# Sparse attention and a rational MLP on one core: how q, k and V are cast, loaded and ordered

## What is computed

```
scores = (q @ k^T) / sqrt(64)
mask_local   = (rel >= 0) & (rel < 32)                 # heads 0-3, rel = query - key
mask_strided = (rel >= 0) & (key % 32 == query % 32)   # heads 4-7
attn = softmax(where(mask, scores, -1e9)); y = attn @ v
x = y.transpose(0, 2, 1, 3).reshape(4608, 512)
h = x @ w_in                                           # 512 -> 2048
g = (a0 + a1 h + a2 h^2 + a3 h^3) / (1 + |b0| |h| + |b1| h^2 + 1e-6)
out = g @ w_out                                        # 2048 -> 512, float32
```

## Time and profile before

| | |
|---|---|
| median of 3 runs | 556.41 us (552.62 to 563.49) |
| profiled execution | 551.65 us, its span 549.9 us |
| busy time PE / DVE / ACT | 353.3 / 345.4 / 255.2 us of the span |
| DMA packets | 176,959, of them 164,384 under 512 B; 60.35 MB |
| software queue q0 (POOL: casts, weights, stores) | 43,840 packets, 27.79 MB |
| hardware queue q1 (SP: loads, transposes) | 133,088 packets, 32.11 MB |

### The profile page before, as it was taken

One profiled execution on the slowest core, in us unless ns is written; L12 is line 12 of the kernel. 1 busy time (PEld: TensorE's weight loads), 2 busy tenths in 40 slices (PEclk: granted clock), 3 DMA queues, 4 the chain that ended last, 5 costly groups with the idle time before them and its releaser, 6 DMA issues.

```text
span 549.9 us, 7027 instructions
## 1 busy us (share of the span) xinstructions
PE 353.3 (64%) x2993; PEld 162.9 (30%) x3040; DVE 345.4 (63%) x286; ACT 255.2 (46%) x249; POOL 95.9 (17%) x104
## 2 busy tenths in 40 slices
PE   0010123355662996898479677999998769988763
PEld 0000112113221442444134333344443323333221
DVE  2000013012885795899449758799998996999920
ACT  0010001021735473666707516768847865788500
POOL 9400000050041061514301600010020110100100
PEclk9999999995955797998859967999999989999888
DMA  9999992799299999999994986442261211010101
GB/s 133 119 91 101 184 137 58 131 176 92 46 164 160 160 164 186 194 185 175 186 121 88 161 163 138 87 104 63 61 139 31 60 62 39 38 39 19 57 29 49
DMA packets 176959, 60.35 MB, mean 110 GB/s; under 512 B 164384, under 2 KB 173600, under 8 KB 176416
## 3 DMA queue, kind: packets, MB, share of 16 engines
q1 hardware_dynamic: 133088, 32.11, 40.9%
q0 software_dynamic: 43840, 27.79, 37.5%
HBM read 42.83 MB, written 25.95 MB: 125 GB/s over the span
## 4 chain that ended last, share of the span: by engine, by line
DVE 31%; PE 22%; DMA 16%; SPq 14%; ACT 10%; issue 5%; POOL 0%; DVEq 0%; POOLq 0%
PE ps_h L649 10%; DMA ptL<-pL 8%; PE ps_out L691 7%; SPq L433 6%; DVE u L668 6%; DVE z L676 4%; DMA xt<-xs 4%; SPq L442 4%; DMA xs<-xS 3%; DVE z L674 3%; DVE h L678 3%; ACT u L671 3%; DVE u L666 3%; ACT u L669 3%; DVE z L664 3%
## 5 line engine op out<-in xcount | busy, mean ns | idle before, releaser
L691 PE MATMUL ps_out<-Wout,h 128*128 128x512 bf16 x557 | 144.0, 410 | 24.5 <-ACT os L696 19.3
L649 PE MATMUL ps_h<-xt,Win 128*128 128x512 bf16 x548 | 137.7, 396 | 27.1 <-DMA xt<-xs 12.7
L653 ACT ACTIVATE h<-ps_h 128x512 bf16<-128x512 f32 x144 | 84.9, 597 | 79.8 <-PE ps_h L649 79.8
L691 PEld LDWEIGHTS ps_out<-Wout,h 128*128 128x128 bf16 x576 | 57.0, 104 | 101.5 <-ACT os L696 23.2
L649 PEld LDWEIGHTS ps_h<-xt,Win 128*128 128x128 bf16 x576 | 50.7, 101 | 96.5 <-ACT h L653 32.2
L702 POOL DMA_DIRECT2D out_dram<-os x36 | 37.1, 1121 | 241.1 <-ACT os L696 230.5
L669 ACT ACTIVATE u<-u,consts 128x4096 bf16<-128x4096 bf16 x18 | 66.7, 3706 | 17.2 <-DVE u L668 17.0
L389 POOL DMA_DIRECT2D lq<-in_q_dram x16 | 37.4, 2381 | 206.4 <-DMA vL<-v 205.6
L671 ACT ACTIVATE u<-u 128x4096 bf16<-128x4096 bf16 x18 | 65.1, 3619 | 0.0
L696 ACT ACTIVATE os<-ps_out 128x512 f32<-128x512 f32 x36 | 21.5, 597 | 62.3 <-PE ps_out L691 62.2
L389 POOL DMA_DIRECT2D lk<-in_k_dram x16 | 46.7, 3005 | 0.0
(11 more groups left out here) (41 smaller groups left out, 352.7 us busy)
## 6 DMA issues: line engine op xcount, KB each, us to landing
out_dram<-os POOLq DMA_DIRECT2D x36, 256.0 KB, 3.3
v<-in_v_dram POOLq DMA_DIRECT2D x8, 576.0 KB, 12.1
vL<-v SPq DMA_DIRECT2D x32, 96.0 KB, 3.3
lq<-in_q_dram POOLq DMA_DIRECT2D x16, 144.0 KB, 12.1
lk<-in_k_dram POOLq DMA_DIRECT2D x16, 144.0 KB, 13.5
sq<-in_q_dram POOLq DMA_DIRECT2D x8, 288.0 KB, 7.1
sk<-in_k_dram POOLq DMA_DIRECT2D x8, 288.0 KB, 9.6
vS<-v SPq DMA_DIRECT2D x16, 144.0 KB
```

The costliest lines, as they stand in the source:

```text
L649: r = e.matmul(ph.t[:, :], Win[:, kk, f * 128:(f + 1) * 128], xt.t[:, kk, :], start=(kk == 0), stop=(kk == NK1 - 1))
L653: P.op("act", lambda e, f=f, ph=ph, h=h: e.activation(h.t[:, f % G, :], ph.t[:, :], AF.Copy), 0.53, key, r=[ph], w=[h])
L691: r = e.matmul(po.t[:, :], groups[g].t[:, j, m * 128:(m + 1) * 128], Wout[:, kk, :], start=(kk == 0), stop=(kk == NF - 1))
```

## The change

- Casts of q and k for all heads go in natural order into `q16` and `k16`, in rows of 1024 elements, one DMA for four heads (`bulk`). The pair-of-heads layout is gone.
- All heads are loaded by the transposes that put even positions on partitions 0 to 63 and odd ones on 64 to 127. For the local heads four SBUF copies per batch put the other half's data across, so that heads on either half of the partitions have both an even and an odd plane (`PRE`, `halves`, `planes`).
- A local score block of 64 queries becomes two of 32: the even queries and the odd ones. The keys are read from two planes, and the PSUM output is written with a step of two, so that the keys stay in natural order. The queries of a block of 64 then stand in the order even, odd; the mask, the strided heads' xs rows and `xt` follow that order, and ACT puts h back into natural order as it evicts the first layer.
- The local pairs are heads (0, 2) and (1, 3), and the units go L, S, S, L.
- The strided heads' V is cast by POOL straight into SBUF (`vS`); only the local heads' V goes through DRAM.
- casts(1) and the second weights wait for loads of batch 0; casts(b+2) stands behind attention(b) in the list. Keys of the loads and of the MLP are later. The planner doubles a DMA's planned time when another queue is busy.
- xs is written in runs of 2048 elements (4 KB).
- The last chunk's four output blocks take four PSUM banks, those of the attention's tiles.

```diff
+                at = max(dmafree[e], t + o.dur)
+                busy = any(v > at for k, v in dmafree.items() if k != e)
+                dmafree[e] = at + o.dma * (2 if busy else 1)
...
-    R_lqT = ring("lqT", 4, [128, S])
-    R_lkT = ring("lkT", 4, [128, S])
-    R_sqT = ring("sqT", 2, [128, SW])
-    R_skT = ring("skT", 2, [128, SW])
+    SC = S // 2
+    SW = HL * SC
+    PRE = 2 * SC
+    QW = 2 * PRE + 2 * SW
+    R_tq = ring("tq", 2, [128, QW])
+    R_tk = ring("tk", 2, [128, QW])
...
+        qs = 64 * jj + 2 * (qi % 32) + (qi % 64) // 32
+        ks = np.maximum(0, 64 * jj - STRIDE) + ki
+        d = qs - ks
...
+    def bulk(s_t, d_t, b, h0, nh, hd, t, key, after):
+        n = nh * S * D
+        c = 1024
+        P.op("pool", lambda e: e.dma_start(
+            bass.AP(tensor=d_t, offset=(b * hd + h0) * S * D, ap=[[c, n // c], [1, c]]),
+            bass.AP(tensor=s_t.tensor, offset=s_t.offset + (b * H + h0) * S * D, ap=[[c, n // c], [1, c]])),
+            2.75, key, w=[t], dma=1.4 * nh / 4, after=after)
+    halves = {t.name: [Tile(t.name + n) for n in "LSX"] for t in R_tq.tiles + R_tk.tiles}
+    def planes(j, idx):
+        if j == 0:
+            return PRE + idx * SC, PRE + SW * 2 + idx * SC
+        return idx * SC, PRE + (2 + idx) * SC
...
-        local(0)
-        bulk(q, sq, HL, T_sqk[b])
-        bulk(k, sk, HL, T_sqk[b])
-        bulk(v, vs, 0, T_v[b])
-        local(1)
+        for n in range(2):
+            for s_t, d_t, t in ((q, q16, T_q[b][n]), (k, k16, T_k[b][n])):
+                bulk(s_t, d_t, b, HL * n, HL, H, t, key, after)
+            if n == 0:
+                bulk(v, vs, b, 0, HL, HL, T_v[b], key, after)
+        vS = vS_of[b] = R_vS.next()
+        for x in range(2):
+            P.op("pool", lambda e, x=x: e.dma_start(
+                vS.t[64 * x:64 * x + SB, :, :, :].rearrange("t h g d -> t h (g d)"),
+                bass.AP(tensor=v.tensor, offset=v.offset + ((b * H + HL) * S + 8 * x) * D,
+                        ap=[[16 * D, SB], [S * D, HL], [1, 8 * D]])),
+                1.0, key, w=[vS], dma=0.6, after=after)
...
-        key = b * 576 - 700
+        key = b * 576 - 20 if b else -700
...
+        tq, tk = R_tq.next(), R_tk.next()
+        for n in range(2):
+            for t, d_t, dt_ in ((tq, q16, T_q[b][n]), (tk, k16, T_k[b][n])):
+                hf = halves[t.name][n]
+                hf.new()
+                P.op("sp", lambda e, t=t, d_t=d_t, n=n: e.dma_start_transpose(
+                    t.t[:, PRE + n * SW:PRE + n * SW + SW],
+                    d_t[b, HL * n:HL * n + HL, :, :].rearrange("h (c two) d -> (h c) (two d)", two=2)),
+                    1.3, key + 2 * n, r=[dt_], w=[hf], dma=1.5)
+        for t, z in ((tq, halves[tq.name][2]), (tk, halves[tk.name][2])):
+            z.new()
+            for x in range(2):
+                d0 = 0 if x else PRE + 2 * SW
+                s0 = 2 * PRE if x else PRE
+                P.op("sp", lambda e, t=t, x=x, d0=d0, s0=s0: e.dma_start(
+                    t.t[64 * x:64 * x + 64, d0:d0 + PRE], t.t[64 - 64 * x:128 - 64 * x, s0:s0 + PRE]),
+                    0.5, key + 1, r=[halves[t.name][0]], w=[z], dma=0.3)
...
-        for kind, idx in (("L", 0), ("S", 0), ("L", 2), ("S", 2)):
+        for kind, idx in (("L", 0), ("S", 0), ("S", 2), ("L", 1)):
...
+                        for qp in range(2):
+                            p0 = 64 * (jj % 2) + 32 * qp
+                            for j in range(2):
+                                even, odd = planes(j, idx)
+                                off = 64 * j * QW
+                                r = e.matmul(pst[p0:p0 + 32, j, KW * (jj // 2):KW * (jj // 2) + KW].rearrange(
+                                                 "p (c k) -> p k c", k=2),
+                                             bass.AP(tensor=tq.t, offset=off + (even, odd)[qp] + 32 * jj,
+                                                     ap=[[QW, 64], [1, 32]]),
+                                             bass.AP(tensor=tk.t, offset=off + even + c0,
+                                                     ap=[[QW, 64], [odd - even, 2], [1, KW // 2]]),
+                                             start=False, stop=True, skip_group_check=True)
...
-                bass.AP(tensor=xs, offset=(b * S + par) * 256, ap=[[16 * 256, SB], [2 * 256, NBK], [1, 256]]),
+                bass.AP(tensor=xs, offset=(b * S + 32 * par) * 256, ap=[[64 * 256, SB // 4], [8 * 256, 4], [1, 8 * 256]]),
...
-        base = c * CH + 1150
+        base = c * CH + 1500 if c else 1000
...
-                P.op("act", lambda e, f=f, ph=ph, h=h: e.activation(h.t[:, f % G, :], ph.t[:, :], AF.Copy),
+                P.op("act", lambda e, f=f, ph=ph, h=h: e.activation(
+                    h.t[:, f % G, :].rearrange("p (j c k) -> p j k c", k=2, c=32),
+                    ph.t[:, :].rearrange("p (j k c) -> p j k c", k=2, c=32), AF.Copy),
...
-        base = c * CH + 1900
+        base = c * CH + 2250
+        last = [R_ps.next(), R_ps.next()] if c == NCH - 1 else None
         for m in range(CH // 128):
-            po = R_po.next()
+            po = last[m // 2] if last else R_po.next()
+            pot = po.t[:, m % 2, :] if last else po.t[:, :]
...
     casts(0)
     weights_in()
-    casts(1)
-    weights_out()
     nxt = 0
     st = loads(0)
+    casts(1, after=st["ops"])
+    weights_out(st["ops"])
     for b in range(B):
         cur = st
         if b + 1 < B:
             st = loads(b + 1)
+        xl = attention(b, cur)
         if b + 2 < B:
             casts(b + 2, after=st["ops"])
-        xl = attention(b, cur)
         gather(b, xl)
```

More of the change, by code:

```diff
@@ L380, in casts @@
+    def planes(j, idx):
+        if j == 0:
+            return PRE + idx * SC, PRE + SW * 2 + idx * SC
+        return idx * SC, PRE + (2 + idx) * SC
     def casts(b, after=()):
         key = b * 576 - 1500 if b > 1 else -1e5 + 3e4 * b
-        T_lqk[b][0].new()
-        T_lqk[b][1].new()
-        T_sqk[b].new()
+        for n in range(2):
+            T_q[b][n].new()
+            T_k[b][n].new()
         T_v[b].new()
[L387 to L392, removed]
@@ L418, in weights_out @@
                 w_out[512 * j:512 * j + 512, :].rearrange("(a p) n -> p a n", p=128)),
-                3.0, -4e4, w=[T_wout], dma=5.4)
+                3.0, -4e4, w=[T_wout], dma=5.4, after=after)
     def loads(b):
-        key = b * 576 - 700
+        key = b * 576 - 20 if b else -700
         st = {}
[L425 to L435, removed]
+        tq, tk = R_tq.next(), R_tk.next()
+        for n in range(2):
+            for t, d_t, dt_ in ((tq, q16, T_q[b][n]), (tk, k16, T_k[b][n])):
[13 more added lines that the diff above has]
+                    0.5, key + 1, r=[halves[t.name][0]], w=[z], dma=0.3)
+        hq, hk = halves[tq.name], halves[tk.name]
+        st["TL"] = [hq[0], hk[0], hq[2], hk[2]]
+        st["TS"] = [hq[1], hk[1]]
         vl = R_vL.next()
-        VB = (b * H) * S * D
+        VB = (b * HL) * S * D
         P.op("sp", lambda e: e.dma_start(
@@ L446, in loads @@
         st["vl"] = vl
[L447 to L456, removed]
+        st["vs"] = vS_of[b]
+        st["q"], st["k"] = tq, tk
+        st["ops"] = [vl.w[-1], hk[0].w[-1]]
         return st
@@ L478, in score @@
                     for jj in range(NQ):
[L479 to L482, removed]
[L483 to L484 removed]
+                        c0 = max(0, 32 * jj - 16)
+                        for qp in range(2):
[10 more added lines that the diff above has]
+                                             start=False, stop=True, skip_group_check=True)
                     return r
[L486 removed]
+                P.op("pe", score, 1.4, key, r=[T_c] + st["TL"], w=[sc])
                 flat = pst[:, :, 0:W].rearrange("p a (r c) -> p a r c", c=KW)
@@ L690, in mm @@
                         kk = g * G + j
-                        r = e.matmul(po.t[:, :], groups[g].t[:, j, m * 128:(m + 1) * 128], Wout[:, kk, :],
+                        r = e.matmul(pot, groups[g].t[:, j, m * 128:(m + 1) * 128], Wout[:, kk, :],
                                      start=(kk == 0), stop=(kk == NF - 1))
```

53 lines of the change are left out of this document (19 added, 34 removed).

## The result

The changed kernel takes 517.36 us (median of 4 runs, 514.78 to 520.31) against 557.48 us (4 runs, 552.62 to 563.49) for the kernel before: ratio 0.931, 95% interval 0.921 to 0.941. That is 40 us saved where 76 were forecast; the time lies inside the forecast range. The profiled execution took 515.17 us, its span 513.4.

What follows compares the result with a forecast made beforehand. VectorE was taken as the bound, kept idle early by SP's small packets waiting behind the casts' backlog. Prelude 95, stretch 363, tail 16.6 and 1.8 make 476, times 1.0086: 480 us, range 444 to 530.

Steps and rivals of the forecast that it cites:

- A burst keeps its bytes but loses 4608 small packets. I take 90% use: Stretch from VectorE's first to last MLP instruction: VectorE use rises from 84.5% to 90%, 386.6 to 363 us, -24.
- Eight first-layer tiles, 32 matmuls at 0.23 us ... near 10 us: 95: End of prelude: chunk 0's first-layer matmuls and an eviction take near 10 us, VectorE's first MLP instruction at 95 us.
- Queue starved still: Rival: bursts keep their bytes and SP waits as long; prelude 118, stretch 387, tail 16.6, scaled 528 us; 15%.
- 4600 more are 9 us: 85: Prelude: attention(0)'s packets left after the second burst (over at 76 us) take 9 us, to 85 us.
- The sign as written: Sign of being right, on SP: no issue over 10 us after the first 40 us.
- Signs of being wrong: `ptL` of 10 us and more in every burst, local score over 3, first `z` after 115, VectorE waiting as often.
- Local scores: TensorE in attention: 18 matmuls (0.40 us) become 36 at 1.45 us, 15 us more in the stretch, hidden; 0 taken.
- the last rival: Rival: the 36 score matmuls don't overlap, 8.3 us a unit, 7.9 more; scaled total 578 us; 4%.
- Eviction: First-layer eviction writing every other bf16 stays at 597 ns, cost 0; doubled, ScalarE 297 us, under VectorE's 326; at most +15.
- SP's four copies: Loads per batch: four small copies more against fewer issues, taken as level; 0, or 24 us if loads never run ahead.
- POOL's wait in front of the strided-V cast: Strided-V cast of batch b+2 waits for batch b's last strided AV; three output tiles cover it, 0 taken.
- Tail: After VectorE's last instruction: four banks leave 32 matmuls, 9.0 us in place of 16.5, -7.5; tail 16.6 us.

Runs made afterwards that it cites:

- run without the later bursts: Changed kernel without bulk casts of q, k and local V for batches 2 to 7, their loads reading batches 0 and 1: 487.94 us, ratio 0.8878.
- old keys: Changed kernel with the MLP keys of the kernel before (1150 and 1900 for 1500 and 2250): 529.78 us; with smaller packets and PSUM-side step too, 512.85 us.
- held burst: Changed kernel with casts(2) waiting until VectorE's first z of chunk 0: 520.73 us, ratio 0.950.
- gather first: Changed kernel with loads(1), and casts(2) after them, waiting until chunk 0 of xt is gathered: 520.87 us, ratio 0.9507.
- one later burst: Spread version, but all of a later batch's casts behind the first attention unit of the batch before: 516.18 us, ratio 0.9414.
- Spreading: Changed kernel with later batches' casts in four pieces, each behind an attention unit of the batch before, loads(b+1) behind attention(b): 500.84 us, ratio 0.903.

## Why the forecast was right in sign and 39 us short

In the profiled executions the forecast was 476 us and the measurement 515.17: of the difference 22.9 us are in the prelude, 13.4 in the stretch, 2.5 in the tail.

**The step that failed** is the size of the later cast bursts. In the stretch it reads "A burst keeps its bytes but loses 4608 small packets. I take 90% use"; in the prelude, "Eight first-layer tiles, 32 matmuls at 0.23 us ... near 10 us: 95" takes no burst in its time at all. Measured were 85.7% and 21.7 us (96.16 to 117.92). In the run without the later bursts these are 91% (327.5 of 360.64 us) and 11.1 (96.52 to 107.62), and the sum is 484.9 of span against 474.6 forecast. That run has an order of its own, so that not all of this need be the bursts' doing.

The rival "Queue starved still" describes the stretch a little better (387 us, against 363 forecast and 376.35 measured). That its prelude of 118 is the measured 117.92 is luck: the second burst was over at 65 us, and what took the time was the third burst and the step below. Its premise, that the queues advance packet for packet, doesn't hold in the third burst. From 90 to 106 us:

```profile
q0 software_dynamic: 458, 1.68, 77.3%
q1 hardware_dynamic: 2046, 0.50, 25.3%
```

q1 moves 128 packets per us beside this burst, against 483 from 65 to 90 us with q0 empty. The forecast took fewer cast packets for a smaller burst. But a quarter of the packets did not shorten the transposes: from first z on, the longest `ptL` and `xt<-xL` took 14.6 and 12.9 us from issue to landing, 13.4 and 10.8 in the kernel before, and 7.6 and 3.5 without the later casts. The run with 50% more packets, in the changed kernel's order, agrees; with the old keys the question stays open. In the changed kernel it is bytes in a lump, not packets, that delay `ptL`, `ptS` and the gather.

**A second step was mis-sized**, "4600 more are 9 us: 85". It counts packets and takes the time of SP's issues at nothing. q1 then moved 12,084 packets in 25 us, 483 per us, and that this is near the 509 of the sum is chance. SP was issuing for 19.9 of the 20.4 us from 69.77 us on (the timeline of SP above), 1.2 to 1.5 us for each transpose, and in the middle the DMA engines were mostly idle:

```profile
74.50:83.00 8.50, 0.00 (x0) 0.00 (x0) 0.00 (x0) 0.00 (x0) 0.00 (x0) 1.00 0.37 73
```

11.05 us of these issues are loads(1), which SP's list puts ahead of the gather's end and which the step leaves out. The first MLP matmul came at 96.16 us, not 85, although the steps before had been 11 us pessimistic (second burst over at 65 us, not 76): the step took 31 us in place of 9. Putting the gather first, which cures this alone, made first z 28 us earlier and the whole slower.

**And the sum itself was too simple.** It adds prelude and stretch as if a shorter prelude ended the kernel earlier. Four runs moved first z by 7 to 28 us forward without a gain, since attention was no earlier: its last strided unit came at 389.19 us (held burst), 391.5 (gather first) and 399.67 (one later burst), for 384.81 in the changed kernel, and at 381.77 with gather first and no later casts, for 359.57 without the later casts alone. In the changed kernel this unit is 61 us earlier than before (384.81 for 445.92), but three chunks stand behind it in the fixed order instead of two: the last `h` ends 109.5 us after it, 79.8 before. In the first two runs and the one without later casts it is again 107 to 109 us. What ends earlier is what lets attention end earlier, or shortens what stands behind it. Spreading did mostly the second: the unit came 2.3 us earlier (382.53), and 99.4 us followed, as VectorE had done 11.6 us more work by then. There the earlier first z was worth its 10 us.

What sets attention's own pace once the bursts are gone was not settled. The granted clock is higher without them too (0.89 and 0.99 in the windows of the stretch, 0.85 and 0.95 in the changed kernel); no run separates it from them.

Point by point:
- Direction, and the gain from holding back: right. loads(0) had landed at 35.1 us (forecast 46), and the longest SP issue of the whole span is 7.55 us, where it was 19.15. The sign as written, no issue over 10 us after the first 40, tells nothing: the kernel before has none there either (the longest 9.55).
- Signs of being wrong: first z after 115 us came true (117.92), and `ptL` took over 10 us in three later bursts (issued at 90.18, 211.7 and 286.10 us).
- Local scores: 0.59 us at the higher clock level against 1.45 forecast. The timeline of PE:

```profile
199.68 0.59 PE L498 MATMUL ps_s<-tk,tq 64*32 64x96 bf16 x36
```

  That is 16 ns a matmul, against 22 before. Half the queries and every other PSUM word cost 0.2 us a unit; the last rival is gone. The Trainium skill's sentence (Advanced Engine Details and Errata, Memory Cachelines) that a non-contiguous PSUM pattern slows matmuls isn't borne out here, by these 16 and 22 ns; the same 36 matmuls with output in runs were not measured.
- Eviction: forecast at 597 ns, measured 743, hidden as the bound said (VectorE waits 9.2 us for `h` in the stretch). The bound's 297 us was added up wrong: the stretch before has 136 evictions, 80.1 us, so that doubled they bring ScalarE from 240 to 320 us, still under VectorE's 326.
- SP's four copies, taken as level: they waited 0.7 us for a transpose, once.
- POOL's wait in front of the strided-V cast: 0 taken, 1.9 us measured, once.
- Tail: 32 matmuls took 7.08 us (forecast 9.0), but what follows them, taken as in the kernel before, grew. The timeline:

```profile
491.98 2.29 DVE L700 TENSOR_TENSOR h<-z,u 128x4096 bf16<-128x4096 bf16 x1 [1.38 <-ACT u L693]
...
494.33 7.08 PE L715 MATMUL ps_s<-Wout,h 128*128 128x512 bf16 x32 [1.41 <-DVE h L700]
...
502.34 0.54 POOL L726 DMA_DIRECT2D out_dram<-os  x1 [1.19 <-ACT os L720]
```

  From the issue of the last store to the end of the span it is 11.06 us, 6.73 before (543.17 to 549.9), though the store's data have moved by 505 us. In the traces it goes with the set of casts and with nothing else that was changed: 11.0 us in the eight kernels with the changed kernel's casts, spread ones among them, 10.1 in the three with smaller packets, 8.6 in the two without later casts, 6.7 in the three with the casts of the kernel before (four stores per block, 12.8, apart). Why, no run shows. So the tail of 16.64 us without later casts meets the forecast's 16.6 by chance: 2 us less for the matmuls, 2 more behind them.

## What to carry to other kernels

A transfer that an engine waits for was delayed here by the bytes queued beside it when it was issued, however few packets they came in. Cutting a bulk transfer into pieces and tying each to a step of the work that it runs beside won 3 points; smaller packets, or one burst elsewhere, won nothing. Before adding up stages, ask which chain sets the end: an earlier start of one engine was worth nothing in four runs, where the stage that feeds it later wasn't earlier too, and paid only where less work was left behind that stage. When counting a queue's backlog, read the issue order of its engine and count everything that stands ahead, the next batch's loads too, and count the time of the issues as well as the packets. A part that does nothing beside one order of the work can be worth something beside another, as smaller packets and the PSUM-side step together were with the old keys.

## What the runs showed of the hardware

- ScalarE's eviction of 512 elements from PSUM to SBUF took 743 ns when it wrote every other bf16, 597 when both sides were in runs, and 598 when it read PSUM out of order and wrote in runs.
- 36 small matmuls (64x32 by 64x96) that write every other 4-byte PSUM word took 0.59 us, 18 (64x64 by 64x96) that write in runs 0.40, both at the higher clock level.
- 10,176 and 15,296 packets for the same 27.8 MB on the software queue gave the same time (0.931 and 0.9325).
- Two DMA queues with work advanced packet for packet in two windows before (1373 and 1374, 3062 and 3000 packets), but not beside casts of large packets, where q0 moved 458 packets (1.68 MB) and q1 2046 (0.50 MB) in 16 us.
- A DMA transpose of the gather held SP for about 1.25 us (five in 6.34), and from 74.5 to 83 us, with SP issuing throughout, the DMA engines were 37% busy.
- The time between the issue of the last 256 KB store and the end of the span was 6.7, 8.6, 10.1 or 11.0 us between kernels whose last store is the same, by which casts they issue earlier.
